# Layer two's first product, chunk pairs 0 and 1: from classic quarters to seven products in blocks

## The reference

```python
h = x @ w_in;  solu = h * softmax(h);  x = (layernorm(solu) * g_ln) @ w_out     # d_ff 1024
h = x @ w2_in                                                                    # 512 -> 2048
g = max(h, 0) ** 2
out = g @ w2_out                                                                 # 2048 -> 512
```

## Time and profile before

| what | value |
|---|---|
| median of 3 runs (lowest, highest) | 470.56 us (470.23, 470.58) |
| time of the profiled execution | 471.22 us |
| its span | 469.4 us |
| granted TensorE clock | 0.999 |
| PE busy | 459.4 us (98% of the span) |
| DVE, ACT, POOL busy | 352.7, 236.3, 125.9 us |

### The profile page before, as it was taken

How to read it: one execution, slowest core, us unless ns; L and a number is a source line. 1 busy time by engine, 2 the same in 40 slices (tenths; PEclk the granted TensorE clock), 3 DMA queues, 4 the chain that set the end, 5 groups by cost and what they waited for, 6 DMA issues and landing times.

```text
span 469.4 us, 8094 instructions
## 1 busy us (share of the span) xinstructions
PE 459.4 (98%) x2970; PEld 403.1 (86%) x2970; DVE 352.7 (75%) x592; ACT 236.3 (50%) x605; POOL 125.9 (27%) x175
## 2 busy tenths in 40 slices
PE   8989999999999999999999999999999999999997
PEld 6657787787778888788999999999988899888997
DVE  2899889988898898975682666666799997442792
ACT  3678777756765765644362222213545355222450
POOL 2356333051302311522245765553000000000000
PEclk9999999999999999999999999999999999999999
DMA  7921234543654773565401110111520011100011
GB/s 224 323 67 56 67 68 137 168 122 82 172 156 106 187 183 98 137 138 132 109 17 47 45 34 13 46 45 46 182 88 0 1 47 45 46 0 1 22 46 68
DMA packets 61471, 41.92 MB, mean 89 GB/s; under 512 B 28344, under 2 KB 50104, under 8 KB 61432
## 3 DMA queue, kind: packets, MB, share of 16 engines
q1 hardware_dynamic: 60664, 40.74, 31.2%
q10 hardware_dynamic: 768, 0.66, 0.5%
HBM read 30.38 MB, written 11.01 MB: 88 GB/s over the span
## 4 chain that ended last, share of the span: by engine, by line
PE 87%; DVE 4%; POOL 3%; DMA 2%; ACT 1%; issue 1%; SPq 1%; POOLq 0%; DVEq 0%
PE h_ps L1959 11%; PE wo_ps L1999 11%; PE wo_ps L2245 7%; PE score_ps L2161 7%; PE h_ps L2193 5%; PE score_ps L2193 5%; PE score_ps L2214 5%; PE wt_ps L2214 5%; PE h_ps L2214 5%; PE wo_ps L2193 4%; PE wt_ps L2193 4%; PE wo_ps L1921 3%; PE score_ps L1887 2%; PE wt_ps L2245 2%; PE score_ps L2245 2%; PE wo_ps L2024 2%
## 5 line engine op out<-in xcount | busy, mean ns | idle before, releaser
L1220 ACT ACTIVATE ring<-g 128x512 fp32r<-128x512 f32 x66 | 40.8, 630 | 50.8 <-PE h_ps L2214 12.0
L1673 DVE TENSOR_TENSOR g_low<-g,ring 128x512 fp32r<-128x512 f32 x66 | 45.0, 690 | 27.6 <-ACT ring L1220 26.9
L956 ACT ACTIVATE prob<-sm,nbias 128x132 f32<-128x132 f32 (+1 forms) x96 | 37.7, 394 | 4.7 <-DVE nbias L1334 4.0
L1959 PE MATMUL h_ps<-w_hi,xT_hi 128*128 128x512 f32 x88 | 35.2, 401 | 1.2 <-DVE xT_lo L1443 0.9
L1999 PE MATMUL wo_ps<-wo_hi,lnT_hi 128*128 128x512 f32 x88 | 36.1, 411 | 0.0
L2245 PE MATMUL wo_ps<-wst,ring 128*128 128x256 f32 x192 | 35.3, 283 | 0.0
L1999 PE MATMUL wo_ps<-wo_hi,lnT_lo 128*128 128x512 f32 x88 | 34.9, 397 | 0.0
L1999 PE MATMUL wo_ps<-wo_lo,lnT_hi 128*128 128x512 f32 x88 | 34.4, 391 | 0.0
L1959 PE MATMUL h_ps<-w_hi,xT_lo 128*128 128x512 f32 x88 | 34.4, 391 | 0.0
L1959 PE MATMUL h_ps<-w_lo,xT_hi 128*128 128x512 f32 x88 | 34.3, 390 | 0.0
L879 POOL TENSOR_TENSOR w_lo<-w_raw,w_hi 128x512 fp32r<-128x512 f32 x16 | 22.1, 1384 | 41.9 <-ACT w_hi L1184 41.9
(11 more groups left out here) (250 smaller groups left out, 1382.3 us busy)
## 6 DMA issues: line engine op xcount, KB each, us to landing
u_dram<-uT SPq DMA_DIRECT2D x18, 256.0 KB, 3.3
lnT_raw<-u_dram SPq DMA_DIRECT2D x36, 128.0 KB, 2.9
w_raw<-w_in SPq DMA_DIRECT2D x16, 256.0 KB, 3.3
V<-v SPq DMA_DIRECT2D x12, 256.0 KB, 3.3
x_dram<-x SPq DMA_DIRECT2D x44, 64.0 KB, 2.2
out<-y SPq DMA_DIRECT2D x11, 256.0 KB, 2.0
k_raw<-kT SPq DMA_DIRECT2D x20, 132.0 KB, 2.8
q_raw<-qT SPq DMA_DIRECT2D x20, 128.0 KB, 2.8
```

What stands on the lines that cost most here:

```text
L956: nc.scalar.activation(prob[:, h, seen(n)], sm[:, h, seen(n)], ACT.Exp, bias=nbias[:, h:h + 1], scale=-1.0 if alone(n) else SCALE, accum_o ...
L1220: nc.scalar.activation(item_high(n), item_raw(g, n), ACT.Copy).then_inc(item_rounded, 1)
L1673: nc.vector.tensor_tensor(item_raw(g_low, n), item_raw(g, n), item_high(n).bitcast(F32), ALU.subtract).then_inc(item_split, 1)
L1959: done = mm(h_ps[:, cols], xs[:, c, :], ws[:, c, cols], start=(c == 0 and k == 0), stop=(c == MC - 1 and k == 2))
```

## The change

Pairs 0 and 1 are now also multiplied by seven products, for each pass m by itself, with both pairs in one group: `block_product(m, n)`, 2 pairs x 2 halves x 3 = 12 matmuls of 384 columns, n = 0 to 6, m = 0 and 1. That is 14 groups of 12 in place of 16. The order of the products is new (M_FIRST, M_SECOND, M_SIXTH, M_FIFTH, M_SEVENTH, M_FOURTH, M_THIRD). M_FIRST of pass 0 stands ahead of the projection of tile 10 (two quarters stood there), M_SECOND behind the transposes of tile 11, the rest behind the projection of tile 11. ACT keeps partial sums (`keep_first`, `keep_second`, `keep_third`) and the DVE adds corners (`add_corner`). The weights of pairs 0 and 1 now need their sums too, so POOL's `sum_w2` is cut in an upper and a lower half and runs for these pairs as well; chunk pair 1 is loaded early, to a place of its own. All x operands have a place of their own now (B12 is no longer an operand). The core of the diff:

```diff
+BLOCK_PRODUCTS = ((A11, B11, 0, True), (A12, B21, 1, True), (S2, T2, 0, False), (S1, T1, 1, True),
+                  (S3, T3, 0, False), (A22, T4, 2, True), (S4, B22, 1, False))
+EARLY_PARTS = ((0, 0), (1, 0), (0, 1), (1, 1), (0, 2), (0, 3), (1, 2), (1, 3))
...
@@ SP
                 if t == NT - 3:
                     load_w2(0)
+                    load_w2(1)
             load_x2T(1, TPB, TPB + QH3, x2T_loaded[1])
             store_x2(NT - 3)
             sp.wait_ge(lnT_split, len(LN_PARTS) * (NT - 1))
-            load_w2(1)
+            store_x2(NT - 2)
             load_w2(2)
-            store_x2(NT - 2)
+            load_w2(3)
             load_x2T(1, TPB + QH3, NT - 1, x2T_loaded[2])
             store_x2(NT - 1)
             load_x2T(1, NT - 1, NT, x2T_end_loaded)
...
             def load_w2(j):
 
                 if since(j, 2):
-                    sp.wait_ge(w2_split, w2_parts_before(j - 1))
+                    sp.wait_ge(w2_split, w2_parts_until(j - 2, 3))
...
@@ POOL
-            split_w2(0)
+            split_w2(0, 0)
+            sum_w2_upper(0)
+            split_w2(1, 0)
+            sum_w2_upper(1)
+            sum_w2_lower(0)
+            sum_w2_lower(1)
             inverse_std(NT - 1)
-            split_w2(1)
+            for j, part in EARLY_PARTS[CLASSIC:]:
+                split_w2(j, part)
             for j in range(CLASSIC, NJ):
-                sum_w2(j)
-                split_w2(j)
+                sum_w2_upper(j)
+                sum_w2_lower(j)
+                for part in range(4):
+                    split_w2(j, part)
...
@@ ACT
+            def keep_first(m):
+                act.wait_ge(multiplied, multiplied_before(m) + M_FIRST + 1)
+                nc.scalar.copy(block_corner(m, 1, 0), block_pair(m, 0)).then_inc(block_kept, 1)
+            def keep_second(m):
+                act.wait_ge(multiplied, multiplied_before(m) + M_SIXTH + 1)
+                nc.scalar.copy(block_corner(m, 0, 1), block_pair(m, 0)).then_inc(block_kept, 1)
+            def keep_third(m):
+                act.wait_ge(multiplied, multiplied_before(m) + M_SEVENTH + 1)
+                act.wait_ge(block_added, len(CORNERS) * m + 1)
+                nc.scalar.copy(block_corner(m, 1, 0), block_pair(m, 0)).then_inc(block_kept, 1)
...
-            round_w2(0)
+            round_w2(0, 0)
+            round_w2(1, 0)
+            round_w2(0, 1)
             hidden_exp(NT - 1)
             hidden_sum(NT - 1)
-            round_x(0, B12)
             for part in range(len(LN_PARTS)):
                 round_lnT(NT - 2, part)
-            drain(0)
+            keep_first(0)
+            round_w2(1, 1)
+            round_x(0, T2)
             round_x(0, B22)
-            drain(1)
-            round_w2(1)
+            for j, part in EARLY_PARTS[2 * CLASSIC:]:
+                round_w2(j, part)
             for part in range(len(LN_PARTS)):
                 round_lnT(NT - 1, part)
-            drain(2)
             round_x(0, T1)
-            round_x(0, T2)
             round_x(0, T3)
+            round_x(0, T4)
             act.wait_ge(x2_done, NT)
             round_x(1, B11)
+            keep_second(0)
             round_x(1, B21)
...
+            keep_third(0)
+            keep_first(1)
+            round_x(1, T2)
+            round_x(1, T1)
+            round_x(1, T3)
+            keep_second(1)
+            round_w2(2, 0)
             round_x(1, B22)
...
             round_x(1, T4)
+            round_w2(2, 1)
+            keep_third(1)
...
@@ DVE
+            def add_corner(m, i):
+                r, h = CORNERS[i]
+                product, bank, added_to = ((M_SECOND, 1, (1, 0)), (M_FIFTH, 1, (1, 0)), (M_FOURTH, 2, (1, 0)), (M_THIRD, 1, (0, 1)))[i]
+                dve.wait_ge(multiplied, multiplied_before(m) + product + 1)
+                dve.wait_ge(block_kept, 3 * m + (1, 3, 3, 2)[i])
...
-            split_x(0, B12)
+            sum_x(0, T1)
             normalize_hidden(NT - 1)
-            split_x(0, B22)
+            sum_x(0, T2)
+            split_x(0, T2)
             square_x2(NT - 2)
             for part in range(len(LN_PARTS)):
                 split_lnT(NT - 1, part)
-            sum_x(0, T1)
-            sum_x(0, T2)
             sum_x(0, T3)
+            sum_x(0, T4)
+            add_corner(0, 0)
+            split_x(0, B22)
+            split_x(0, T1)
+            split_x(0, T3)
+            split_x(0, T4)
             square_x2(NT - 1)
             split_x(1, B11)
             split_x(1, B21)
...
+            add_corner(0, 1)
+            add_corner(0, 2)
+            add_corner(0, 3)
             sum_x(1, T1)
             sum_x(1, T2)
             sum_x(1, T3)
             split_x(1, T2)
+            add_corner(1, 0)
+            split_x(1, T1)
             split_x(1, T3)
...
+            split_x(1, B22)
             split_x(1, T4)
+            add_corner(1, 1)
+            add_corner(1, 2)
+            add_corner(1, 3)
...
@@ PE, block_product(m, n), its waits
+                pe.wait_ge(xc_split[m][xk], 1)
+                if n == M_FIRST and m == 0:
+                    pe.wait_ge(merged, merges(NT))
+                elif n == M_SECOND and m == 1:
+                    pe.wait_ge(block_added, 3)
+                elif n == M_SIXTH:
+                    pe.wait_ge(block_kept, 3 * m + 1)
+                elif n == M_FIFTH:
+                    pe.wait_ge(block_added, len(CORNERS) * m + 1)
+                elif n == M_SEVENTH:
+                    pe.wait_ge(block_kept, 3 * m + 2)
...
+                elif n == M_THIRD:
+                    pe.wait_ge(block_added, len(CORNERS) * m + 2)
```

More of the change, by code:

```diff
@@ L67 @@
 NP = len(PRODUCTS)
+BLOCK_PRODUCTS = ((A11, B11, 0, True), (A12, B21, 1, True), (S2, T2, 0, False), (S1, T1, 1, True),
+                  (S3, T3, 0, False), (A22, T4, 2, True), (S4, B22, 1, False))
+M_FIRST, M_SECOND, M_SIXTH, M_FIFTH, M_SEVENTH, M_FOURTH, M_THIRD = range(NP)
+CORNERS = ((0, 0), (1, 1), (1, 0), (0, 1))
+GATES = tuple((m, r) for m in range(PASSES) for r in (1, 0))
+EARLY_PARTS = ((0, 0), (1, 0), (0, 1), (1, 1), (0, 2), (0, 3), (1, 2), (1, 3))
 P_FIRST, P_SECOND, P_CORNER, P_THIRD, P_LOWER, P_LEFT, P_RIGHT = range(NP)
@@ L710, in _ @@
             load_x2T(1, NT - 1, NT, x2T_end_loaded)
-            for j in range(3, NJ):
+            for j in range(4, NJ):
                 load_w2(j)
@@ L1169, in round_x, with round_w2 @@
                     act.wait_ge(x2T_end_loaded, MOVES)
-                if k == T4:
-                    act.wait_ge(multiplied, len(QUARTERS) * CLASSIC * (s + 1))
+                if s == 0 and k in (T1, T4):
+                    act.wait_ge(w2_split, w2_parts_before(CLASSIC))
+                elif s == 1 and k in (T2, T3):
+                    for read in (B21, B22, T3):
+                        act.wait_ge(xc_split[0][read], 1)
                 nc.scalar.activation(x_hi(s, k)[:, :, :], x_combination(s, k), ACT.Copy).then_inc(xc_rounded[s][k], 1)
-            def round_w2(j):
+            def round_w2(j, part):
                 act.wait_ge(w2_loaded[j % 2], 32 * (j // 2 + 1))
@@ L1294, in _ @@
                 if j + 1 < NJ:
-                    round_w2(j + 1)
+                    for part in range(4):
+                        round_w2(j + 1, part)
             round_item(6)
@@ L2144, in _, with block_product @@
             last_step()
[L2147 to L2163 removed]
+            def block_product(m, n):
+                wk, xk, bank, opens = BLOCK_PRODUCTS[n]
+                pe.wait_ge(xc_split[m][xk], 1)
[9 more added lines that the diff above has]
+                    pe.wait_ge(block_kept, 3 * m + 2)
+                elif n == M_FOURTH and m == 0:
+                    pe.wait_ge(x2_squared, NT)
+                elif n == M_FOURTH:
+                    pe.wait_ge(block_kept, 3)
+                elif n == M_THIRD:
+                    pe.wait_ge(block_added, len(CORNERS) * m + 2)
+                for j in range(CLASSIC):
+                    if m == 0:
+                        pe.wait_ge(w2_split, w2_parts_until(j, (0, 0, 1, 1, 2, 2, 3)[n]))
+                    for c in range(2):
+                        for k in range(3):
+                            ws, xs = ((w2_hi, xc_hi), (w2_hi, xc_lo), (w2_lo, xc_hi))[k]
+                            last = mm(block_pairs[m][bank][:, j, 0:TH], ws[j][:, wk, c, :], xs[m][xk][:, c, :],
+                                      start=(opens and c == 0 and k == 0), stop=(c == 1 and k == 2), skip_group_check=True)
+                last.then_inc(multiplied, 1)
@@ L2247, in seven_part @@
                 done.then_inc(item_done, 1)
-            pe.wait_ge(merged, merges(NT))
-            quarter(0)
-            quarter(1)
+            block_product(0, M_FIRST)
             project(NT - 2, 0, 24)
             transpose_ln(NT - 1)
-            quarter(2)
+            block_product(0, M_SECOND)
             project(NT - 1, 0, 24)
-            for n in range(3, 16):
-                quarter(n)
+            for n in range(M_SIXTH, NP):
```

(3 more changed lines are left out.)

162 lines of the change are left out of this document (67 added, 95 removed).

## The result

The changed kernel takes 474.16 us (median of 5 runs, 474.02 to 475.59) against 470.57 us before (470.23 to 471.64): ratio 1.0080, 95% interval 1.0061 to 1.0098. It is slower by 3.6 us where 0.3 us was forecast, and lies outside the forecast range. Of the five executions four, with a mean granted clock of 0.996, took 474.02 to 474.49 us, and the one at 1.000 took 475.59. The profiled execution took 474.10 us with a span of 472.0 us.

A forecast was written before the change was run, and what follows sets the result against it. TensorE was taken to bound the stage, with no idle time between matmuls. Terms -4.17 + 1.5 + 0.35 + 2.2 + 0.5 gave +0.4, by absolute times +0.3, taken as 470.9 us median; range 468.6 to 472.7.

The forecast's parts named there:

- Part 2: Head of the order, up to project(11): POOL's new work costs nothing, tile 11 normalized at 212.5, project(11) wanted at 216.82.
- Part 4: M_SEVENTH of pass 0: waits for ACT's copy behind an x load queued after two weight loads, +0.35 us.
- Part 6: M_FOURTH of pass 1: waits for the split of T4 beside POOL's split of chunk 2, +0.5 us (0.1 to 1.1).
- Part 1: TensorE's block products: 16 groups become 14, 24 matmuls at 0.1737 us removed, -4.17 us, all on the path.
- Part 3: project(11): late because T2's sum and ACT's roundings stand ahead of tile 11's rounding, a stall of +1.5 us.
- Part 5: M_SIXTH of pass 1: waits for T2, through tile 11's sums, splits, squares, store and load, +2.2 us.
- The rival of the high end: Tile 11's way: DVE pays all of POOL's sums, T2 and M_FOURTH(1) later, +1.85 on top of +0.3, 472.7 us; chance 0.26.

The follow-up runs named there:

- e1: Changed kernel with POOL's splits of the early weight parts waiting until tile 11 is normalized; 474.06 us, ratio to before 1.0066.
- e8: e7 without POOL's wait, so its early splits again run beside the normalization of tile 11; 470.18 us, ratio 0.9984.
- e2: Changed kernel with M_SECOND of pass 0 computed twice, unneeded work where TensorE idled; 474.08 us, ratio 1.0076.
- e5: Changed kernel with SP issuing pass 1's third x load ahead of the loads of chunks 2 and 3; 473.64 us, ratio 1.0049.
- e10: e7 with tile 11's squares put back behind the splits of T3 and T4; 471.23 us, ratio 1.0001.
- e7: e6 with e3's order, tile 11's rounding and squares earlier, second kept copy ahead of pass 1's first rounding; 468.44 us, ratio 0.9948.
- e3: Changed kernel with ACT rounding pair 2's first two weight parts behind pass 1's last x operands and third kept sum; 473.45 us, ratio 1.0061.
- e6: Changed kernel with e1's wait on POOL and e5's earlier x load together; 471.19 us, ratio 1.0007.
- e4: Changed kernel with M_SIXTH of pass 0 ahead of tile 11's projection, its kept copy right behind tile 11's rounding; 474.78 us, ratio 1.0085.
- e9: e5 with M_SECOND of pass 0 computed twice, filling the idle time with unneeded work; 472.51 us, ratio 1.0030.

## Why the prediction was wrong

The mechanism was named: the saved matmuls turn into waits for tile 11. The step that failed first is the price of the normalization of tile 11 beside POOL's new splits: 1.00 us in Part 2, 2.94 measured. Three more followed: the x load in Part 4 (4.76 us, measured 6.17), the last splits in Part 6, and the clock, a loss that was not on the list. Where a point in time is compared below, it is counted from the start of the stage, which came 0.48 us earlier than before.

- **Part 1 was right.** 0.174 us from matmul to matmul, 4.17 us removed.
- **Part 2 was wrong in one point.** POOL's work ahead of `inverse_std(11)` cost nothing (it waited 2.85 us for the moments), but the work behind it did. I gave the normalization its old 1.00 us although POOL's new splits start with it. The sentence on the Trainium skill said that GpSimd contends with VectorE instructions in a 2-port mode too, and I kept it out of the sum and priced it at 0.5 us. The 0.5 has no working and no row behind it. It took 1.94 us. In its place the 0.6 us that I had added for T2's sum were not needed: POOL was done by then.
- **Part 3 was mis-sized:** +1.5 forecast, +2.26 measured. e1 and e8 show the normalization as the cause of the excess, and of the 0.23 us in the transposes. **What the idle time can do to the clock was missing:** +1.68 us in the projection. It was put at nothing without a reason; the table of before has the clock at 0.999, as the mean of the whole execution. e2 shows that these 1.68 us alone cost the kernel nothing, since Part 4's load was as late.
- **Part 4 came out right by chance:** +0.35 forecast, +0.27 measured. The x load took 6.17 us, not 4.76, with 1 MB of weights ahead of it (4.75 again in e5), and its first issue, at 222.67, was some 1.4 us later than booked, nearly all of that because the store of tile 10 came late (217.39), itself behind the late normalization. ACT's copy was late by 2.8 us in all; TensorE was late by as much for its own reasons, the longer stall and the slow clock. e2 shows the tie. I had booked the wait of the second weight load, but not what its data do to the load behind it.
- **Part 5 was too large as a stall,** 2.2 forecast, 0.78 measured, because TensorE came later. What set it was not tile 11's load but the add of the corner behind M_THIRD: the sum follows that add at 238.05 without a wait for a transfer. The 2.0 us of contention added to the DVE's splits were about 1.1 (two splits at 1.50 and 1.49). Where TensorE is on time and the squares are late (e10), the load is what holds it, as forecast; with early squares (e7) it is the add again.
- **Part 6 was mis-sized:** +0.5 forecast, +1.57 measured. POOL's two splits cost the DVE 1.6 us over both of its last splits; e3 removes them.

In the stage the terms add up so: +0.3 was forecast, and 0.23 (transposes), 0.76 (Part 3), 1.68 (clock), 0.19 (Part 4 and the restarts around it), 1.07 (Part 6) and 0.25 (restarts) came on top, less 1.42 (Part 5), about 2.8 us in all.

The rival of the high end, contention at full price with tile 11's way as its place, is nearest to what happened, but it had its place wrong and ended at 472.7.

## What to carry to other kernels

Cost a moved operation of VectorE also by what GpSimd does beside it, where the trace of before has no such pair: here one wait on POOL was worth 1.7 us. Where two chains end together, mend both before judging either: e1 alone gave nothing, e5 alone 0.5 us, e6 with both 3 us. Look at where a profiled execution lies among the others before reading its largest wait: that of e6 came from one slow transfer. A saving of TensorE's work at full occupancy is worth its full size only when everything that feeds it moves forward by the same time; check every load behind another in the queue and every copy behind a wait.

## What the runs showed of the hardware

- Beside two splits on GpSimd (2.73 us) that began 0.08 us earlier, VectorE's two fp32 tensor_scalar from SBUF to SBUF took 2.94 us, 1.51 each in place of 0.54; with GpSimd idle, 1.00 for both (e1, e6, e7). GpSimd lost little there. Where VectorE had begun first, GpSimd lost: 1.98 in place of 1.30, beside a sum of VectorE that began 0.14 us earlier and kept its 0.95. In the rows where both lose they take turns by whole instructions: POOL's sum ends at 225.65, VectorE's split, begun at 224.97, ends 0.82 us later at 226.47, and POOL's next sum, begun at 225.73, 0.59 us after that. Alone such a split takes 0.95 and such a sum 0.74. So in these rows the one that came later waited until the other's instruction was done. VectorE's split of lnT with one input in PSUM took 0.42 us at 218.38, in the midst of POOL's splits (217.02 to 221.63), no longer than the 0.46 each that those of its size took with POOL idle.
- By the rule in the Trainium skill, GPSIMD Engine Reference, section 8 Key points, GpSimd contends with VectorE instructions in a 2-port mode or with two SBUF inputs; the trace agrees, with 1.94 us for the two tensor_scalar and 0.47 and 1.11 us for the last two x splits, which have two SBUF inputs.
- After idle times of 2.08 us (the changed kernel), 2.41 us (e1), 2.53 us (e4) and 1.81 us (e3) TensorE's granted clock went from its upper level, 2.4 GHz, to the lower one, 1.2 GHz, and back; matmuls of 512 columns came every 0.43 us in place of 0.23 meanwhile, which cost 1.68 us in the changed kernel. After 1.77 us (e2), 2.08 us (e3, ahead of the projection), 2.11 us (e5), 2.28 us (e10) and 2.81 us (e6) in other profiled executions it did not. So in these runs the length of the idle time did not decide it. Filled with matmuls that nobody needs, the gap ahead of the projection left the clock at 0.999 or more in all 12 executions of e9, against 4 of 12 in e5.
- A transfer can be slow in one execution only: the parts of tile 11's load landed 2.2 to 2.4 us after their issue in most profiled executions, and one of them after 3.4 (e2), 3.5 (e4) and 4.4 us (e6).
